# The front of a chunked delta-rule attention reordered ahead of two mixtures of experts

## The chip, the cores and the metric

One core of one Trainium2 chip runs the whole program. The metric is the device time of one execution in microseconds (us); for the kernel before it is 2411.12 us, the median of three runs (2405.57 to 2415.29).

## The reference, cut to what matters

```python
# attention: q, k, v (4, 8, 768, 48), beta (4, 8, 768)
k_n = k / (norm(k, axis=-1) + 1e-6)
for t in range(768):
    y[:, :, t] = einsum('bhd,bhde->bhe', q[:, :, t], state)
    v_old = einsum('bhde,bhd->bhe', state, k_n[:, :, t])
    state = state + beta_t * einsum('bhd,bhe->bhde', k_n[:, :, t], v[:, :, t] - v_old)
x = y.transpose(0, 2, 1, 3).reshape(3072, 384)
# first mixture: 8 experts, all tokens through all of them, weights P
P = exp(x @ w_gate - max); 8 times: rows and columns normalised
out = sum_e P[:, e] * (relu(x @ w1[e]) @ w2[e])     # 384 -> 1024 -> 384
# second mixture: every token goes to one expert, by argmax of normalised scores
```

## The kernel before, in words

The program has three stages on the core: the attention with expert 0 of the first mixture mixed in, experts 1 to 7 of the first mixture over all tokens, and the second mixture over sorted tokens. The change touches only the first stage.

The attention is done in 12 chunks of 64 positions, for 32 heads at once (16 head columns `j` on each half of the partitions, 64 matmuls a product). For each chunk the kernel needs two products that do not depend on the recurrent state: `gram`, keys times keys, and `mix`, keys times queries. ScalarE copies a mix out of PSUM (`copy_m`, L588) and GpSimd masks it (`mask`, L505). VectorE scales a gram by the inverse key norms and beta (`scale`, L858), and SyncE stores it to HBM (`store_a`). The norms come from `kn` loads in six parts of two chunks (`squares_of` L584, `reduce_part` L828, `norms` L835 to L850, done for the first two chunks and then for the other ten).

The triangular inverse of a pair of chunks is solved on VectorE by substitution. `load_blocks(n)` (L339) brings the diagonal 32 by 32 blocks of pair n back from HBM with eight DMAs, `solve` (L876, L879) runs 31 row steps of two instructions, `transpose_blocks` on ScalarE (L595) makes the transpose `sr`, and `store_inverse` (L343, L345) writes `sx` and `sr` to HBM. `load_inverse(c)` (L358, L362, L365) reads them back for chunk c in the layout that TensorE needs, after a wait for those stores.

The recurrence per chunk then runs on TensorE in this order, with ScalarE and VectorE steps between: `cross` (L1224), `corner` (L1232), `write_values` (L1184, psA), `outputs` (L1248, L1184, L1256), `transpose_y` (L1206), `scores` (L1213), and `keys_state` (L1184, psA) for the next chunk. `high_x` (L621, L623) on ScalarE and `low_x` (L513) on GpSimd split the transposed chunk into a high and a low part, `X`. Expert 0 works from these: block k of 96 is `block_hidden(k)` (L1273) and, two steps later, `block_give` (L1290); 8 blocks belong to one chunk.

The order of all this is written out by hand. After a straight prologue every engine runs the same loop over steps s = 0 to 103. Step s holds block s - 8, and lists of step numbers say when each piece of each chunk is issued: `AT_KS`, `AT_X`, `AT_O`, `AT_W`, `AT_Y`, `AT_T`, `AT_SC` for `keys_state`, `cross`, `corner`, `write_values`, `outputs`, `transpose_y` and `scores`; `AT_SOLVED[n]` is the step in which VectorE ends the solve of pair n. From chunk 2 on all lists have a period of 8 steps. In one step TensorE issues its block first, then keys_state, transpose, scores, cross, corner, write_values and outputs, as far as they fall in this step. ScalarE issues the `Relu` of the block (L666), then the copies of the chain, then `high_x`, and only after it `transpose_blocks`. Every engine takes its instructions strictly in this written order. SyncE issues all of the stage's DMAs in one queue, and a wait on it holds everything behind it.

In the kernel before, `cross` of chunk 4 is in step 28, and `AT_SOLVED[2]` is 22:

```python
AT_KS = [None, 4] + [10 + KF * (c - 2) for c in range(2, NC)]
AT_X = [0, 6] + [t + 2 for t in AT_KS[2:]]
AT_T = [t + 1 for t in AT_Y]                      # AT_Y: AT_KS + 7
AT_SOLVED = [None, 7] + [16 * n - 10 for n in range(2, NG)]
```

## Time and profile before

| | before |
|---|---|
| median of 3 runs | 2411.12 us |
| the profiled execution | 2415.61 us |
| its span | 2413.8 us |
| TensorE busy in the span | 93% |
| TensorE busy, us 0 to 203.7 | 104.4 us |
| TensorE busy, us 203.7 to 500 | 295.7 us |
| mean granted clock of TensorE over the span | 0.954 |

The profile page gives for each engine its busy time and share, then the span in 40 slices. In the chain of waits the work that ended last is followed back from the end; the timeline lists instructions with the idle time before them and its releaser. In a windows table a stretch of the span has one row: its length, the busy time of each engine with instruction counts, the granted TensorE clock (1.00 is 2.4 GHz, 0.50 is 1.2 GHz), the busy share of the DMA engines and the rate in GB/s. The stage of the change ends about us 551 of the span; the stages behind it are not edited.

### The profile page before, as it was taken

How to read it: one execution, taken by the hardware profiler on the slowest of the kernel's cores; microseconds unless marked ns; L12 is line 12 of the kernel's file. 1: busy time of each engine (PE TensorE's matmuls, PEld its weight loads, DVE VectorE, ACT ScalarE, POOL GpSimd, SP SyncE). 2: the span in 40 equal slices, each digit the busy share in tenths (PEclk: the TensorE clock that was granted, in tenths of full speed). 3: DMA queues.
4: the chain of work that ended last, by engine and by line, in shares of the span. 5: the costliest groups of instructions: out<-in, count | busy, mean ns of one | idle time of the engine just before them, and what ended most of it. 6: DMA issues, size and time to landing. Idle time of an engine off the chain costs nothing.

```text
span 2413.8 us, 43024 instructions
## 1 busy us (share of the span) xinstructions
PE 2251.8 (93%) x18100; PEld 2089.6 (87%) x18100; DVE 1015.2 (42%) x1787; ACT 611.5 (25%) x1019; POOL 168.4 (7%) x133
## 2 busy tenths in 40 slices
PE   3279999999999999999999999999999996899998
PEld 3279999998999998999899899989999886899998
DVE  4556666335332332323233232333333325666664
ACT  2123333222111111111111111111111122466664
POOL 1231100100000000000000000000000000222221
PEclk7589999999999999999999999999999997899999
DMA  8564443331000000000000000000000012665651
GB/s 233 119 163 104 111 111 90 102 125 46 7 27 1 27 23 5 27 1 27 1 27 27 1 27 1 27 20 8 1 1 1 14 40 63 222 239 201 234 201 61
DMA packets 152487, 166.92 MB, mean 69 GB/s; under 512 B 82956, under 2 KB 113840, under 8 KB 152322
## 3 DMA queue, kind: packets, MB, share of 16 engines
q1 hardware_dynamic: 147458, 152.21, 20.8%
q0 software_dynamic: 4864, 12.20, 1.4%
q8 instruction: 141, 2.31, 0.4%
q14 instruction: 24, 0.20, 0.0%
HBM read 138.42 MB, written 28.71 MB: 69 GB/s over the span
## 4 chain that ended last, share of the span: by engine, by line
PE 91%; DVE 4%; DMA 2%; issue 2%; SPq 1%; ACT 1%; POOL 0%; POOLq 0%; DVEq 0%; ACTq 0%
PE psA L1369 21%; PE psH L1384 15%; PE psB L1369 8%; PE psB L1384 7%; PE psY L1384 7%; PE psY L1478 7%; PE psH L1273 4%; PE psY L1290 4%; PE psA L1465 3%; PE psB L1465 3%; PE psA L1184 3%; PE psB L1256 1%; PE psB L1248 1%; PE psY L1184 1%; DVE products L876 1%
## 5 line engine op out<-in xcount | busy, mean ns | idle before, releaser
L1369 PE MATMUL psA<-X,wh 128*128 128x512 f32 x1440 | 460.5, 401 | 18.1 <-issue 14.0
L1007 DVE SCALAR_TENSOR_TENSOR hl<-psA,hh 128x512 fp32r<-128x512 f32 x240 | 166.0, 692 | 656.6 <-ACT hh L708 656.6
L708 ACT ACTIVATE hh<-psA 128x512 fp32r<-128x512 f32 x240 | 143.8, 599 | 876.9 <-PE psA L1369 876.9
L1369 PEld LDWEIGHTS psA<-X,wh 128*128 128x128 f32 x1440 | 273.8, 193 | 65.9 <-issue 19.7
L1369 PE MATMUL psA<-X,wl 128*128 128x512 f32 x720 | 290.3, 403 | 0.0
L1384 PE MATMUL psH<-wh,hh 128*128 128x384 f32 x672 | 229.0, 341 | 0.0
L1384 PE MATMUL psH<-wh,hl 128*128 128x384 f32 x672 | 227.4, 338 | 0.0
L1384 PE MATMUL psH<-wl,hh 128*128 128x384 f32 x672 | 226.1, 337 | 0.0
L1007 DVE SCALAR_TENSOR_TENSOR hl<-psB,hh 128x512 fp32r<-128x512 f32 x96 | 66.5, 693 | 278.6 <-ACT hh L708 278.6
L1369 PE MATMUL psB<-X,wh 128*128 128x512 f32 x576 | 179.2, 392 | 0.0
L1131 DVE TENSOR_TENSOR vl<-vs,vh 128x768 fp32r<-128x768 f32 x152 | 145.0, 957 | 58.2 <-ACT vh L745 56.6
L1369 PEld LDWEIGHTS psA<-X,wl 128*128 128x128 f32 x720 | 138.5, 192 | 30.3
L708 ACT ACTIVATE hh<-psB 128x512 fp32r<-128x512 f32 x96 | 57.5, 599 | 344.0 <-PE psB L1369 344.0
L745 ACT ACTIVATE vh<-vs 128x768 fp32r<-128x768 f32 x152 | 127.3, 840 | 15.2 <-DMA vs<-v_d 15.2
L1384 PEld LDWEIGHTS psH<-wh,hh 128*128 128x128 f32 x672 | 126.9, 189 | 0.0
L1384 PEld LDWEIGHTS psH<-wl,hh 128*128 128x128 f32 x672 | 126.6, 188 | 0.0
L1384 PEld LDWEIGHTS psH<-wh,hl 128*128 128x128 f32 x672 | 126.2, 188 | 0.0
L1369 PEld LDWEIGHTS psB<-X,wh 128*128 128x128 f32 x576 | 106.7, 188 | 17.7
L1273 PE MATMUL psH<-X,wh 128*128 128x256 f32 x576 | 115.8, 297 | 2.2 <-DVE hlA L886 2.2
L1384 PE MATMUL psB<-wh,hl 128*128 128x384 f32 x336 | 114.4, 341 | 0.0
L1369 PE MATMUL psB<-X,wl 128*128 128x512 f32 x288 | 114.0, 396 | 0.0
L1384 PE MATMUL psB<-wl,hh 128*128 128x384 f32 x336 | 114.0, 339 | 0.0
(236 smaller groups left out, 4290.1 us busy)
## 6 DMA issues: line engine op xcount, KB each, us to landing
vs<-v_d SPq DMA_DIRECT2D x38, 768.0 KB, 6.2
vs<-v_d SPq DMA_DIRECT2D x19, 1536.0 KB, 12.1
ws<-w_d SPq DMA_DIRECT2D x28, 768.0 KB, 6.1
a_scratch<-an SPq DMA_DIRECT2D x12, 512.0 KB, 3.9
kq<-kn_d SPq DMA_DIRECT2D x6, 768.0 KB, 8.6
pk<-kT_d SPq DMA_DIRECT2D x24, 192.0 KB, 4.3
pq<-qT_d SPq DMA_DIRECT2D x24, 192.0 KB, 5.5
vn<-vn_d SPq DMA_DIRECT2D x12, 384.0 KB, 4.5
```

Source lines behind the costliest of these rows:

```text
L708: act.activation(hh[kk % 3][:, :], ps_h[kk % (2 if last else 3)], ACT.Relu).then_inc(hh_ready, 1)
L745: act.activation(piece(to, q), piece(src, q), ACT.Copy).then_inc(vh_ready, 1)
L876: dve.tensor_tensor(pv, sa[n % 2][:, s + 1:BS, s:s + 1].to_broadcast([P, rows, cols]), sx[:, s:s + 1, 0:cols].to_broadcast([P, rows, cols] ...
L1007: dve.scalar_tensor_tensor(hl[b][:, :], ps_h[bank], 0.0, hh[b][:, :].bitcast(F32), ALU.max, ALU.subtract).then_inc(hl_ready, 1)
L1131: dve.tensor_tensor(piece(to, q), piece(src, q), piece(high, q).bitcast(F32), ALU.subtract).then_inc(vl_ready, 1)
L1184: mm = pe.matmul(ps[g * C:g * C + M, j, at:at + W], lhsT[g * C:g * C + K, j, 0:M], rhs[g * C:g * C + K, j, 0:W], start=True, stop=True, sk ...
L1273: mm = pe.matmul(ps_b[k % 2], a[half][:, c, col], X[:, u, b, c, :], start=(n == 0), stop=(n == 3 * KC - 1))
L1290: mm = pe.matmul(ps_u[i], a[k % 4][:, i * P:(i + 1) * P], b[half][:, f % FB, :], start=(f == 0 and n == 0), stop=(f == KF - 1 and n == 2))
L1369: mm = pe.matmul(to, a[half][:, c, col], X[:, 2 * g:2 * g + 2, b, c, :], start=(n == 0), stop=(n == 3 * KC - 1))
L1384: mm = pe.matmul(ps_y[i][:, 0:DM], a[kk % 3][:, q], b[half][:, f, :], start=(f == 0 and n == 0), stop=(f == FB - 1 and n == 2))
L1465: mm = pe.matmul(ps_g[f % 4], a[par][:, c, f * P:(f + 1) * P], b[par][:, c, :], start=(n == 0), stop=(n == 3 * KC - 1))
L1478: mm = pe.matmul(ps_o[s], a[f % 4][:, q], b[par][:, f, :], start=(f == 0 and n == 0), stop=(f == KF - 1 and n == 2))
```

## The change

The edits, all in the first stage:

- Keys and queries for gram and mix are loaded as pairs of chunks (`load_pair`, two DMAs of 48 partitions by two chunks) into three key and three query buffers. All mixes are now done in the prologue; keys of chunks 4 to 11 are loaded a second time for their grams. The keys for chunks 6 and 7 are loaded again after `load_first`, which brings in the first expert's weights.
- The key norms come in three batches: chunks 0 and 1, chunks 2 to 5, chunks 6 to 11.
- The norm of the expert embeddings moves from the start to step 10 (ScalarE) and 11 (VectorE).
- `solve(0)` runs as one uninterrupted stretch on VectorE. On ScalarE all 12 mask copies now stand ahead of `transpose_blocks(0)`.
- Masks, `low_x` and the low half of the first expert's weights move from GpSimd to VectorE; the weights' split moves from the prologue into steps 4 to 9.
- `ts` and `ao` get two buffers; `ao` has its own loader, `load_corner`, and `load_inverse` of both chunks of a pair is issued together.
- The step lists: chunk 1 is done earlier (cross in step 2 and not 6), chunks 2 to 11 are three steps later, `AT_SOLVED` of pairs 2 to 5 is six steps later, pair 1 is solved by step 12 and not 7.

```diff
-AT_KS = [None, 4] + [10 + KF * (c - 2) for c in range(2, NC)]
-AT_X = [0, 6] + [t + 2 for t in AT_KS[2:]]
-AT_W = [2, 8] + [t + 5 for t in AT_KS[2:]]
-AT_Y = [3, 9] + [t + 7 for t in AT_KS[2:]]
+AT_KS = [None, 4] + [13 + KF * (c - 2) for c in range(2, NC)]
+AT_X = [0, 2] + [t + 2 for t in AT_KS[2:]]
+AT_W = [2, 5] + [t + 5 for t in AT_KS[2:]]
+AT_Y = [3, 6] + [t + 7 for t in AT_KS[2:]]
-AT_SOLVED = [None, 7] + [16 * n - 10 for n in range(2, NG)]
+SOLVE_SECOND = [4, 3, 3, 3, 2, 2, 2, 2, 2, 2, 2, 2, 2]
+AT_SOLVED = [None] + [16 * n - 4 for n in range(1, NG)]
+AT_MASK = [None, 2] + [t + 1 for t in AT_KS[2:]]
+AT_SPLIT = {4: (0, 0), 5: (0, 1), 7: (1, 0), 8: (1, 1)}
+AT_EMB = 10
...
# SyncE
+                def load_pair(to, src, m, s):
+                    for g in range(2):
+                        sp.dma_start(to[g * C:g * C + D, :, :, :], src[GR * m:GR * (m + 1), g].rearrange("c d j t -> d c j t")).then_inc(s, 16)
...
-                    for g in range(2):
-                        p0 = g * C + BS
-                        sp.dma_start(aos[p0:p0 + BS, :, :], a_dram[c, p0:p0 + BS, :, 0:BS]).then_inc(s_inv[par], 16)
-                        for k in range(2):
+                    for k in range(2):
+                        for g in range(2):
...
                 load_parts(0)
+                load_pair(kP[0], kT, 0, s_kP[0])
                 sp.dma_start(betas[:, :, :], beta).then_inc(s_beta, 16)
+                load_parts(1)
+                load_pair(qP[0], qT, 0, s_qP[0])
+                load_pair(kP[1], kT, 1, s_kP[1])
+                load_parts(2)
                 sp.dma_start(cst[:, :], consts).then_inc(s_const, 16)
                 sp.dma_start(vns[:, :, :], vn[0]).then_inc(s_vn, 16)
                 for c in range(2):
                     store_a(c)
                 load_blocks(0)
+                sp.wait_ge(s_red, 2)
+                load_pair(qP[1], qT, 1, s_qP[1])
+                load_pair(kP[2], kT, 2, s_kP[2])
+                sp.wait_ge(s_red, 3)
+                load_pair(qP[2], qT, 2, s_qP[2])
+                for m in range(3, PARTS):
                     load_parts(m)
+                for c in range(2):
+                    load_corner(c)
+                store_a(2)
...
+                for m in range(KP, PARTS):
+                    sp.wait_ge(m_done, GR * (m - KP + 1))
+                    if m == KP + 1:
+                        sp.wait_ge(g_done, 4)
+                    load_pair(kP[m % KP], kT, m, s_kP[m % KP])
+                    load_pair(qP[m % KP], qT, m, s_qP[m % KP])
                 sp.dma_start(kns[:, :, :], kn[0]).then_inc(s_kn, 16)
                 halves(kTs, kT, 1, s_kT)
                 halves(qTs, qT, 1, s_qT)
+                sp.wait_ge(m_done, GR * KP + 2)
+                load_pair(kP[0], kT, 2, s_kP[0])
+                store_inverse(0)
+                store_a(3)
+                for c in range(2):
+                    load_inverse(c)
                 load_blocks(1)
+                sp.wait_ge(s_red, PARTS)
+                load_first(0)
+                load_first(1)
+                sp.wait_ge(m_done, NC)
+                load_pair(kP[1], kT, 3, s_kP[1])
+                store_a(4)
+                store_a(5)
                 for s in range(LAST):
+                    if s + 6 < NC:
+                        store_a(s + 6)
+                    if s in (0, 2):
+                        m = 4 + s // 2
+                        sp.wait_ge(g_done, 2 * m - 2)
+                        load_pair(kP[m % 2], kT, m, s_kP[m % 2])
...
-                    if s - 3 in AT_SOLVED:
-                        load_inverse(2 * AT_SOLVED.index(s - 3))
-                    if s - 1 in AT_O[0::2]:
-                        load_inverse(AT_O.index(s - 1) + 1)
+                    if s - 2 in AT_SOLVED:
+                        for par in range(2):
+                            load_inverse(2 * AT_SOLVED.index(s - 2) + par)
+                    if s - 2 in AT_X[0:NC - 2]:
+                        load_corner(AT_X.index(s - 2) + 2)
...
# ScalarE, prologue
                 squares_of(0)
+                root(0)
+                squares_of(1)
+                copy_m(0)
+                squares_of(2)
+                root(1)
+                for c in range(1, 4):
+                    copy_m(c)
+                for c in range(4, NC):
+                    copy_m(c)
+                    if c in (5, 7, 9):
+                        squares_of(3 + (c - 5) // 2)
                 transpose_blocks(0)
+                root(2)
...
# VectorE, prologue
                 reduce_part(0)
+                norms(0)
                 scale(0, psA)
                 scale(1, psB)
+                reduce_part(1)
+                reduce_part(2)
+                norms(1)
+                mask(0)
+                scale(2, psA)
+                solve(0, 0, BS - 1)
+                scale(3, psA)
+                for m in range(3, PARTS):
+                    reduce_part(m)
+                scale(4, psA)
+                scale(5, psH)
+                norms(2)
...
# TensorE, prologue; in step s of the loop then gram(s + 6) after the chain's pieces
                 gram(0, psA)
                 gram(1, psB)
+                mix(0)
                 pe.wait_ge(an_ready, 1)
                 gram(2, psA)
                 pe.wait_ge(an_ready, 2)
+                for c in range(1, 4):
+                    mix(c)
+                pe.wait_ge(an_ready, 3)
+                gram(3, psA)
+                for c in range(4, NC):
+                    mix(c)
+                pe.wait_ge(an_ready, 4)
+                gram(4, psA)
+                pe.wait_ge(mt_copied, NC - 1)
                 gram(5, psH)
```

## Rows read from the trace of the kernel before

**Rows 1.** The page: busy us, share of the span and instructions of each engine.
```profile
PE 2251.8 (93%) x18100; PEld 2089.6 (87%) x18100; DVE 1015.2 (42%) x1787; ACT 611.5 (25%) x1019; POOL 168.4 (7%) x133
```

**Rows 2.** Windows: start:end, length, busy of PE, PEld, DVE, ACT, POOL, clock, DMA.
```profile
0.00:110.90 110.90, 29.39 (x705) 28.80 (x706) 62.41 (x109) 24.61 (x23) 29.05 (x16) 0.64 0.67 178
110.90:176.60 65.70, 51.27 (x1362) 49.64 (x1362) 30.00 (x56) 12.38 (x16) 17.55 (x8) 0.77 0.66 165
176.60:203.70 27.10, 23.70 (x408) 22.59 (x406) 14.30 (x33) 9.16 (x13) 5.61 (x3) 0.87 0.61 155
304.00:500.00 196.00, 195.59 (x3595) 185.31 (x3595) 94.81 (x215) 61.06 (x109) 18.61 (x11) 1.00 0.36 94
```

**Rows 3.** Timeline of the prologue: start, length, engine, line, operation, idle before and releaser.
```profile
22.30 1.47 ACT L584 ACTIVATE kq<-kq 128x1536 f32<-128x1536 f32 x1
90.69 1.94 ACT L595 ACTIVATE sr<-sx 128x1024 f32<-128x1024 f32 x1 [26.04 <-DVE sx L879]
107.74 0.47 SPq L362 DMA_DIRECT2D rs<-r_scratch  x1
110.90 1.92 PE L1224 MATMUL psB<-rs,ao 32*32 32x32 f32 x64 [8.79 <-DMA rs<-r_scratch]
```

**Rows 4.** Windows of short stretches, for the DMA rate and the clock after an idle TensorE.
```profile
3.00:5.00 2.00, 0.00 (x0) 0.00 (x0) 0.00 (x0) 0.00 (x0) 0.00 (x0) 1.00 1.10 402
8.00:12.00 4.00, 4.00 (x94) 4.00 (x92) 0.00 (x0) 0.00 (x0) 0.00 (x0) 1.00 1.04 221
93.00:99.00 6.00, 5.67 (x106) 5.70 (x108) 1.22 (x1) 0.00 (x0) 0.00 (x0) 0.50 1.02 191
555.00:560.00 5.00, 4.79 (x11) 3.80 (x12) 0.06 (x1) 0.58 (x1) 0.00 (x0) 0.50 0.72 212
```

**Rows 5.** Chain of waits in order of time: start, length, piece (step 18 begins at 224.46).
```profile
203.71 1.13 PE psB L1224 x64
224.46 1.27 PE psH L1273 x9
229.09 0.81 PE psB L1206 x6
230.97 1.05 PE psY L1290 x6
235.48 1.13 PE psB L1224 x64
267.25 1.13 PE psB L1224 x64
```

**Rows 6.** Timeline, ScalarE and VectorE, around the inverse of pair 2.
```profile
247.24 2.08 ACT L595 ACTIVATE sr<-sx 128x1024 f32<-128x1024 f32 x1
262.54 0.85 ACT L623 ACTIVATE X<-xf 128x768 fp32r<-128x768 f32 x1
252.64 0.91 DVE L865 MEMSET sx<- 128x1024 f32 x1 [1.89 <-DMA r_scratch<-sr]
```

**Rows 7.** Timeline, SyncE's queue, the same stretch: issue start and length.
```profile
249.34 0.33 SPq L345 DMA_DIRECT2D r_scratch<-sr  x1
249.76 5.71 SPq L339 DMA_DIRECT2D sa<-a_scratch  x8
260.56 0.49 SPq L362 DMA_DIRECT2D rs<-r_scratch  x1
261.09 0.49 SPq L440 DMA_DIRECT2D kn<-kn_d  x1
261.62 0.90 SPq L318 DMA_DIRECT2D qT<-qT_d  x2
262.56 0.88 SPq L318 DMA_DIRECT2D kT<-kT_d  x2
```

**Rows 8.** The solve's tile: count, ns min/median/max of one, start of the first and last.
```profile
L876 DVE TENSOR_TENSOR products<-sa,sx x186: 190/361/2439, 39.6 to 433.2; 128x31 f32<-128x31 f32 x12, 128x60 f32<-128x60 f32 x12, 128x87 f32<-128x87 f32 x12, 128x112 f32<-128x112 f32 x12
L879 DVE TENSOR_TENSOR sx<-sx,products x186: 191/374/1773, 39.8 to 433.4; 128x31 f32<-128x31 f32 x12, 128x60 f32<-128x60 f32 x12, 128x87 f32<-128x87 f32 x12, 128x112 f32<-128x112 f32 x12
```

More of the change, by code:

```diff
@@ L27 @@
 PARTS = 6
-KQ = 4
+BATCH_ENDS = [1, 3, PARTS]
+KP = 3
+NA = 3
 E, F = 8, 1024
@@ L71, in solve_plan @@
     plan, done = {}, 0
-    for s in range(8):
-        n = min(4, BS - 1 - done)
-        plan[s] = (1, done, done + n)
-        done += n
+    for s, k in enumerate(SOLVE_SECOND):
+        plan[s] = (1, done, done + k)
+        done += k
     for n in range(2, NG):
@@ L136, in build @@
         end_dense = top[0]
-        kq = [keep(f"kq{i}", [P, 2 * NJ, D], at=w_at + 4 * 2 * NJ * D * i) for i in range(KQ)]
+        part, pair = 4 * 2 * NJ * D, 4 * GR * NJ * C
+        kq = [keep(f"kq{i}", [P, 2 * NJ, D], at=w_at + i * part) for i in range(PARTS)]
+        qP = [keep(f"qP{i}", [P, GR, NJ, C], at=at) for i, at in enumerate((wl_at + 2 * part, w_at, w_at + pair))]
         fh1 = [keep(f"fh1_{i}", [P, KC, FH], at=wl_at + 4 * KC * FH * i) for i in range(2)]
@@ L153, in build @@
         rs = [keep(f"rs{i}", [P, NJ, C]) for i in range(2)]
-        ts, aos, xx = keep("ts", [P, NJ, BS]), keep("ao", [P, NJ, BS]), keep("xx", [P, NJ, BS])
+        ts, aos = [keep(f"ts{i}", [P, NJ, BS]) for i in range(2)], [keep(f"ao{i}", [P, NJ, BS]) for i in range(2)]
+        xx = keep("xx", [P, NJ, BS])
         zz, ww, st = keep("zz", [P, NJ, D]), keep("ww", [P, NJ, D]), keep("st", [P, NJ, D])
@@ L243, in build @@
         sx_init, sol, sr_ready, inv_out = sem("sx_init"), sem("sol"), sem("sr_ready"), sem("inv_out")
+        s_ao = [sem(f"s_ao{i}") for i in range(2)]
         x_done, x_ready, o_done, r_ready = sem("x_done"), sem("x_ready"), sem("o_done"), sem("r_ready")
@@ L961, in _ @@
                         state(AT_Y.index(s - 1))
+                    if s - 1 in AT_T:
+                        low_x(AT_T.index(s - 1))
                     u = unit_after(s)
@@ L1253, in outputs @@
                     pe.wait_ge(mt_ready, c + 1)
+                    if c == 0:
+                        pe.wait_ge(r_ready, 4)
                     for g, j in heads():
```

297 lines of the change are left out of this document (130 added, 167 removed).

## The prediction

> **What bounds the kernel now.** I read the page first: TensorE is busy for 93% of the span, and no other engine for half of it [rows 1]. The windows say where the other 7% lies that this change can reach. From us 304 to 500, inside the loop, TensorE is busy 195.6 of 196.0 us at full clock; up to us 203.7 it is busy only 104.4 us in three windows, much of it at the low clock (means 0.64, 0.77, 0.87) [rows 2]. So there are two regimes. In the front TensorE waits, and what counts is the chain through DMAs, VectorE and ScalarE. From the second chunk on TensorE sets the end alone: whatever it idles there is added to the time in full, and nothing taken from another engine there is worth anything. I therefore compare one landmark, `cross(2)`, which starts at 203.71 [rows 5], and then ask whether the loop behind it stays free of waits.
>
> The timeline of the prologue shows the old chain: the first squares start at 22.3, because ScalarE stood at the expert embeddings, which are queued behind all the first loads; the solve of pair 0 ends when `sr` starts at 90.7; the last inverse load is issued at 107.7 and `cross(0)` starts at 110.9 [rows 3].
>
> **The front, part by part.** All times are my placement of the new order, with durations of the rows.
>
> *DMA.* A load to all 128 partitions ran at 402 GB/s, one to 48 partitions (keys and queries) at 221, both at a full busy share [rows 4]. The prologue now brings twelve pair loads (0.79 MB each, 3.6 us at 221: 43 us), six norm parts (12 us at 402), three gram stores, eight small block loads, constants and values (some 10 us together) before the last mix can run. With a start of 2.3 us and some 4 us of waits for buffers that is us 71.5 for the last queries. From them: two mixes at the low clock, since TensorE idles before each pair (106 matmuls took 5.67 us there [rows 4], so 64 take 3.4 to 3.7): 79; the copy out of PSUM about 1: 80. The transpose stands behind copy 11 on ScalarE, though the solve ended long before: the blocks are back at 29.5, and 31 steps of 0.36 + 0.37 us [rows 8] make 23 us: 52.6. The clean solve thus gives nothing here; it is the mixes and their loads that are late next. `sr` 1.9 us: 82; its store lands 3.3 us after issue [rows 6, 7]: 85; six loads issued in 3.2 us, the last lands some 3 us after its issue (cross(0) began 3.2 us after it before [rows 3]): `cross(0)` at 91, 20 us earlier than now.
>
> *Behind it* SyncE issues six more inverse loads and eight block loads (8 us), the expert weights (2 us of issue, 3.15 MB, 8.3 us of transfer) and only then the keys of chunks 6 and 7, which move behind the weights in the same queue: they land at 110.5. `gram(6)` stands directly behind `cross(0)` on TensorE, so TensorE idles 17 us there. Half of the gain is gone by this one place.
>
> *Steps 0 to 7* hold six grams, the rest of chunk 0 and all of chunk 1. Before, us 110.9 to 176.6 held the same but seven mixes more and without the last three pieces of chunk 1: 51.3 us busy at a mean clock of 0.77 [rows 2], 39.5 at full clock, less seven mixes of 1.9, plus 8 us for those pieces (a period of 31.8 us less eight blocks leaves 13.2 for a chunk's chain [rows 5]): 34 us of TensorE, 6 us more for two stretches at the low clock, and 9 us of waits (chunk 8's keys behind the store of gram 6: 1; `keys_state(1)` behind `scale(9)` and solve steps on VectorE: 5; write values and scores of chunk 0: 3). The first block starts at 110.5 + 49 = 159.5.
>
> *Steps 8 to 12.* VectorE has ten solve steps, five `low`, half the weight split, `low_x` and the embedding norm: some 15 us against 11 on TensorE. The solve of pair 1 ends at 177.4; `sr` 2.1, store 3.3 (182.7), three issues more and six inverse loads: `cross(2)` at 191.7, after 9 us of idle TensorE. Masks, `low_x` and split on VectorE cost 0 beyond this: GpSimd did them off the path, and in the loop VectorE is busy 95 of 196 us [rows 2]; if that cover were gone, a mask (1.2 us) would be late by its own length.
>
> So cross(2) moves from 203.7 to 191.7: 12.0 us. It also has three more blocks behind it, step 15 and not 12, each 1.27 + 1.05 us [rows 5]: 7.0. **The front gains 19 us.**
>
> **The loop, and what falls due in it.** `AT_SOLVED` moves six steps, the crosses three. Before, pair 2 was solved in step 22 and crossed in 28; now it is 28 and 31. I lay the chain on the clock of step 29, t = 0 at its start. Step 29 is also `AT_T[3]`. In the old order the same three steps are 18 to 20: they start at 224.46, the transpose ends at 229.90, so t = 5.4, and `cross` starts at 235.48, t = 11.0 [rows 5]. ScalarE issues `high_x(3)` before `transpose_blocks(2)`: `xf` and `X` after the transpose end 7.2 us after the step's start (262.54 + 0.85 [rows 6] against 224.46 and a period of 31.77, 256.2). Then:
>
> - `sr`, 2.08 us: 9.3. Its store is issued and lands 3.3 us later (249.34 to 252.64): 12.6 [rows 6, 7].
> - SyncE issues the eight block loads of pair 4 (5.71), then `kn`, `qT`, `kT` (0.49, 0.90, 0.88), all ahead of the inverse loads [rows 7]: 17.9.
> - Six inverse loads, 2.8 to 3.5 us to the issue of the last, 2.5 to land: 23.2 to 23.9.
>
> TensorE stands at `cross(4)` from 11.0: **12.5 us idle**. The same for pair 3. Pairs 4 and 5 have no block loads ahead, and wait for the store to land (12.6) instead: 12.6 + 2.9 + 2.5 = 18.0, **7 us idle** each. Nothing covers this: cross is ahead of the next block in TensorE's order, and the next blocks are ready. Before, the same chain ended with the last load landing at 260.56 + 2.5 = 263.1 against the cross at 267.25 [rows 5, 7]: 4.2 us of slack with six steps' distance, so three steps' distance cannot do. Sum: 2 x 12.5 + 2 x 7 = 39 us.
>
> After an idle stretch the granted clock is 0.50, that is 1.2 GHz, and work goes at half pace: fully so from 93 to 99 after a long wait, and from 555 to 560 after 4 us [rows 4]. Some 6 us at half pace are 3 us lost, five times (pairs 1 to 5): 15 us.
>
> **Sum.** -19 + 39 + 15 = +35 us. The profiled execution took 2415.6 us with a span of 2413.8; with the change 2450.6. It lies 4.5 us above the median of the runs, so the prediction is 2411.1 + 35 = 2446 us. Unknown sizes: the front's 19 may be 5 (each of steps 0 to 7 at the low clock, late weights) to 30; the loop's 39 may be 32 to 46; the clock's 15, 8 to 18 (the row after 4 us of idle shows only 5 us). That is +15 to +55: 2426 to 2466.
>
> **Rivals.**
>
> *The inverse arrives in time* (faster). If ScalarE or SyncE run the pair's chain ahead of TensorE, for instance because the transposes or the loads pass where I see them held, only the front's 19 us are left and perhaps 3 at pair 1: 2411 - 19 = 2392. For it: VectorE has the solve ready before step 29 starts. Against: `high_x(3)` waits for a transpose of the same step, and the slack now is only 4.2 us at twice the distance. It decides from a landing at t = 11 or less, and I find 18 at best. 0.17.
>
> *Pair loads run at the full rate.* The 48-partition rate is the rate of two chunks' pieces of 192 KB; one larger DMA might go at 402. Then each pair takes 2.0 and not 3.6 us, 12 pairs and the late keys 21 us less, of which buffers and half clocks keep 3: +35 - 18 = +17, 2428. Against: these small loads already fill the DMA engines' time, with a busy share of 1.04 [rows 4]. 0.12. The Trainium skill (DMA: Bandwidth & Descriptors, Anatomy of one DMA) gives a DMA a fixed 2.0 us and then bytes by 436 GB/s, which is this rival; the same skill (SBUF — State Buffer, Door 1: The DMA port swizzle) lets 64 partitions in a row reach only half the ports. This trace's 221 against 402 GB/s agrees with the second and not with the first.
>
> *The front gives nothing* (slower still). If the wait at `gram(6)` and the extra VectorE work make cross(2) no earlier than 203.7 less the 7 us of blocks, the gain is 7 or less and the loop's loss stays: +47 to +55, about 2463. For it: 3.15 MB are moved in front of a load on the path. Against: cross(0) at 91 leaves 20 us to spend. 0.13.
>
> **How the numbers follow.** Forecast 0.58 (2426 to 2466), in time 0.17, full rate 0.12, no front 0.13. What can be told from no change is 0.5%, 12 us. Faster by more than that: the first rival, with part of the forecast's low end, 0.18. Within: 0.10. Slower: 0.72. The range runs from 2402 to 2474: it leaves out most of the first rival and the far end of the last, under 0.2 together.
>
> **What would show it.** cross(0) near 91 and cross(2) near 192; gram(6) released by a DMA of keys near 110; in the waits table TensorE L1224 waiting for a DMA of `rs` from `r_scratch` five times, 7 to 13 us each, the two longest for pairs 2 and 3; ScalarE's `sr` directly behind an `X` there; windows of clock 0.50 behind each. If those waits are absent, the prediction is wrong at its root; if cross(2) is after 203, its front is.

## The result and the profile after

The changed kernel takes 2467.94 us (median of four runs, 2462.66 to 2474.41); the kernel before, run beside it, 2412.23 (four runs, 2405.57 to 2415.29). The ratio is 1.0236, 95% interval 1.0203 to 1.0269: slower by 56 us, where 35 were forecast. The profiled span is 2472.5 us against 2413.8, that is +58.7, and the mean granted clock 0.941 against 0.954.

The page after, in its first line (busy us, share, instructions), answers to [rows 1]:

```profile
PE 2280.5 (92%) x18100; PEld 2117.9 (86%) x18100; DVE 1016.1 (41%) x1823; ACT 613.8 (25%) x1020; POOL 106.4 (4%) x106
```

TensorE runs as many instructions in 29 us more of busy time: part of the loss is work at the lower clock. VectorE took over GpSimd's work and is no busier than it was. The windows of the kernel after (columns as in [rows 2]) are cut at its own landmarks: `cross(0)`, the first block, `cross(2)`, and the same inner stretch as before.

```profile
0.00:107.30 107.30, 56.79 (x1153) 55.45 (x1154) 46.53 (x97) 24.84 (x24) 3.55 (x8) 0.70 0.93 201
107.30:191.60 84.30, 56.20 (x1177) 54.56 (x1177) 33.52 (x64) 12.35 (x16) 1.47 (x1) 0.55 0.60 150
191.60:222.50 30.90, 19.47 (x189) 18.05 (x188) 19.09 (x48) 10.01 (x16) 2.16 (x1) 0.90 0.48 117
304.00:500.00 196.00, 165.89 (x2915) 157.35 (x2915) 95.81 (x225) 48.99 (x86) 8.13 (x5) 0.89 0.34 81
```

`cross(0)` comes 3.6 us earlier than before, the first block 15.0 us later, `cross(2)` 18.7 us later. Each of these starts is read from one execution. e8 below has the first stage of the kernel before, unchanged, and there the three start at 108.0, 174.5 and 200.1 and not at 110.9, 176.6 and 203.7, so a difference of some 3 us in them says nothing: the gain at `cross(0)` is not clear of this, the two losses are. The stretch from 304 to 500, full before [rows 2], now has 30 us of idle TensorE and a clock of 0.89. The timeline of the front (start, length, engine, line, operation, idle before and its releaser) answers to [rows 3]:

```profile
36.66 16.54 SPq L366 DMA_DIRECT2D ao<-a_scratch  x4
57.47 0.93 SPq L329 DMA_DIRECT2D kP<-kT_d  x2
70.06 3.68 PE L1235 MATMUL psH<-qP,kP 48*64 48x64 f32 x64 [12.05 <-issue]
107.30 1.92 PE L1284 MATMUL psB<-rs,ao 32*32 32x32 f32 x64 [2.60 <-issue]
129.50 3.68 PE L1235 MATMUL psA<-kP 48*64 48x64 f32 x64 [20.28 <-DMA kP<-kT_d]
222.46 1.92 PE L1284 MATMUL psB<-rs,ao 32*32 32x32 f32 x64 [8.62 <-DMA rs<-r_scratch]
```

The row at 70.06 is mix 6, the one at 129.50 `gram(6)`. How full the DMA engines were ahead of it, in windows of the kernel after (columns as in [rows 2]; the last two figures are their busy share and the rate in GB/s), with one window behind it, for the clock:

```profile
0.00:89.00 89.00, 44.21 (x896) 43.11 (x896) 41.09 (x90) 20.71 (x20) 3.55 (x8) 0.70 0.95 203
60.00:70.00 10.00, 0.00 (x0) 0.00 (x0) 1.75 (x1) 0.46 (x1) 0.00 (x0) 0.50 1.02 181
70.00:80.00 10.00, 7.75 (x157) 7.68 (x159) 0.61 (x1) 3.42 (x3) 0.00 (x0) 0.67 1.03 171
130.00:140.00 10.00, 10.00 (x242) 9.70 (x240) 5.46 (x13) 1.18 (x2) 0.00 (x0) 0.50 0.53 136
```

The loop's waits, from the table of waits (engine, line, awaited thing; us in all, times, longest):

```profile
PE psB L1284 <- DMA rs<-r_scratch: 51.9, 5, 13.4
PE psY L1353 <- DVE y0s L928: 10.4, 8, 2.0
```

and the same table of the kernel before:

```profile
PE psA L1369 <- issue: 14.0, 4, 3.8
PE psB L1224 <- DMA rs<-r_scratch: 8.8, 1, 8.8
```

Before, TensorE waited once for an inverse, at `cross(0)` [rows 3], and at no later cross; now it waits at `cross(2)`, (4), (6), (8) and (10), as forecast: 8.6, 13.4, 13.1, 8.4 and 8.3 us. The stall at `cross(4)`, in the timeline of SyncE, ScalarE and TensorE (columns as above), answers to [rows 6, 7]:

```profile
287.72 0.81 ACT L641 ACTIVATE xf<-psB 128x768 f32<-128x768 f32 x1 [3.47 <-PE psB L1263]
288.56 0.85 ACT L643 ACTIVATE X<-xf 128x768 fp32r<-128x768 f32 x1
289.31 2.00 ACT L611 ACTIVATE sr<-sx 128x1024 f32<-128x1024 f32 x1
291.34 0.32 SPq L357 DMA_DIRECT2D r_scratch<-sr  x1
291.76 4.59 SPq L351 DMA_DIRECT2D sa<-a_scratch  x8
297.86 0.89 SPq L321 DMA_DIRECT2D kT<-kT_d  x2
298.86 0.36 SPq L380 DMA_DIRECT2D rs<-r_scratch  x1
300.85 3.31 SPq L380 DMA_DIRECT2D rs<-r_scratch  x1
306.66 1.92 PE L1284 MATMUL psB<-rs,ao 32*32 32x32 f32 x64 [13.39 <-DMA rs<-r_scratch]
```

Read it as a queue: `sr` stands behind `xf` and `X`, the store behind `sr`, eight block loads and three more transfers behind the store, and only then the inverse. The windows behind it show the price of the clock: 12 us at 0.50 (1.2 GHz) around the stall, then 0.99 (2.4 GHz).

```profile
300.00:312.00 12.00, 5.34 (x78) 5.28 (x79) 0.72 (x3) 1.56 (x3) 0.32 (x1) 0.50 0.91 161
312.00:314.00 2.00, 2.00 (x71) 1.71 (x70) 1.82 (x3) 0.35 (x1) 1.16 (x1) 0.99 0.10 14
```

**The account of the span.** +18.7 us at `cross(2)`. From there to the first product of expert 1 (555.2 before, 636.2 after) +62.3: the four stalls 43.2, the `y0s` waits 10.4, and a rest of 8.7, which is what remains of the half-clock work when the seven us of blocks that already lie ahead of `cross(2)` are taken off. From there to the end -22.3. That last term has nothing to do with attention: no instruction of it was edited.

### The profile page after: what moved, and what is told of

Read it like the earlier page. It is cut to its first block, busy times and chain, and to the rows that moved or that the text cites. A ratio compares the mean times of both kernels' runs of the same rounds, so it can differ in the third digit from the quotient of the medians.

```text
span 2472.5 us, 43060 instructions
## 1 busy us (share of the span) xinstructions
PE 2280.5 (92%) x18100; PEld 2117.9 (86%) x18100; DVE 1016.1 (41%) x1823; ACT 613.8 (25%) x1020; POOL 106.4 (4%) x106
## 4 chain that ended last, share of the span: by engine, by line
PE 85%; DVE 6%; SPq 4%; DMA 2%; issue 2%; ACT 1%; POOL 0%; POOLq 0%; DVEq 0%; ACTq 0%
PE psA L1427 20%; PE psH L1442 14%; PE psB L1427 8%; PE psB L1442 7%; PE psY L1442 7%; PE psY L1536 6%; PE psA L1523 3%; PE psB L1523 3%; PE psA L1235 3%; PE psH L1338 3%; PE psY L1353 3%; PE psH L1235 1%; DVE products L906 1%; PE psB L1311 1%; DVE sx L909 1%
```

## The experiments

Each batch had its own runs of the kernel before; ratios are against those. The medians before differ by up to 2 us between batches, so a difference of two medians of different batches can be off by as much. "Block" and "expert" are the starts, in the profile, of the first block product and of the first product of expert 1.

| Kernel | Median us | Ratio, 95% interval | Block | Expert |
|---|---|---|---|---|
| before | 2412.2 to 2414.2 | 1 | 176.6 | 555.2 |
| after | 2467.94 | 1.0236 [1.0203, 1.0269] | 191.6 | 636.2 |
| e1 before, inverse late | 2464.95 | 1.0218 [1.0199, 1.0238] | 175.9 | 607.9 |
| e2 after, inverse early | 2427.41 | 1.0068 [1.0044, 1.0091] | 190.2 | 589.0 |
| e3 after, keys first | 2463.18 | 1.0198 [1.0177, 1.0219] | 187.0 | 627.2 |
| e5 after, single loads | 2466.09 | 1.0220 [1.0203, 1.0237] | 189.2 | 626.6 |
| e4 after, queues cleared | 2421.30 | 1.0037 [1.0020, 1.0054] | 190.9 | 583.9 |
| e6 after, corner later | 2476.61 | 1.0272 [1.0250, 1.0294] | 192.1 | 635.5 |
| e7 after, four repairs | 2413.06 | 1.0009 [0.9992, 1.0027] | 186.4 | 573.2 |
| e8 before, code shifted | 2391.24 | 0.9917 [0.9895, 0.9938] | 174.5 | 553.2 |
| e9 after, masks on GpSimd | 2481.84 | 1.0285 [1.0263, 1.0307] | 191.2 | 643.0 |
| e10 after, corners late | 2465.22 | 1.0212 [1.0191, 1.0234] | 186.9 | 628.1 |
| e11 e8, inverse first | 2392.55 | 0.9918 [0.9898, 0.9938] | 172.9 | 552.3 |
| e12 e7 varied | 2420.29 | 1.0031 [1.0016, 1.0047] | 182.1 | 576.4 |

**e1: the stalls alone, put into the kernel before.**

```diff
-AT_SOLVED = [None, 7] + [16 * n - 10 for n in range(2, NG)]
+AT_SOLVED = [None, 7] + [16 * n - 7 for n in range(2, NG)]
-                    if s - 3 in AT_SOLVED:
+                    if s - (3 if s < 12 else 2) in AT_SOLVED:
...
```

> The kernel before with one part of the change alone: pairs 2 to 5 are solved three steps before their cross (AT_SOLVED 16n - 7) and their inverse is read one step before it; front, engines of the masks and all else stay as before. Theory (the distance in steps is what costs): TensorE L1224 waits for rs from r_scratch four times, about 13, 13, 8 and 8 us, with 3 us of half-speed work behind each, so the kernel is 48 to 56 us slower than the kernel before: about 2463. Rival (the loop's loss after the change comes from VectorE's added masks and low_x, or from the pair-wise inverse loads): the kernel stays within 5 us of 2412.

Measured 2464.95, 50.8 us above the kernel before of its batch. The table of waits:

```profile
PE psB L1224 <- DMA rs<-r_scratch: 56.9, 5, 14.9
PE psA L1369 <- issue: 14.5, 4, 3.9
```

One of the five waits, 8.0 us, is the old one at `cross(0)`; the late hand-over makes the other four, 14.9, 14.2, 9.9 and 9.9 us, 48.9 in all, and with them nearly as much loss as the whole change brings, without anything of the new front. It keeps the 14.5 us of "issue" gaps, which become e8's question.

**e2: the stalls taken out of the changed kernel.**

```diff
-AT_SOLVED = [None] + [16 * n - 4 for n in range(1, NG)]
+AT_SOLVED = [None, 12] + [16 * n - 6 for n in range(2, NG)]
```

> The changed kernel with AT_SOLVED of pairs 2 to 5 two steps earlier (16n - 6 in place of 16n - 4), nothing else. Theory: the four waits of 7 to 13 us at cross (43.2 us in the trace) go but for a few us, and with them four stretches of half-speed work (3 us each): 2468 - 52 = about 2416, with the wait of 8.6 us at cross(2) left, and the eight waits of 1.3 us for y0s left. Rival (VectorE is too busy in the loop with masks, low_x and solve): solving earlier only moves the wait to hlA, and the time falls by less than 20 us.

Measured 2427.41, 40.5 us less than the changed kernel:

```profile
PE psY L1353 <- DVE y0s L928: 12.3, 8, 2.4
PE psB L1284 <- DMA rs<-r_scratch: 8.3, 1, 8.3
PE psB L1284 <- DVE pm L1023: 6.2, 7, 1.7
```

All four stalls are gone and `cross(2)` keeps its own. Eleven us of the forecast didn't come: half of that is a small new wait at `cross`, for VectorE's copy of the scores. In VectorE's order that copy stands behind solve steps and the mask. At chunk 3 the mask took 2.17 us, against 1.22 in the changed kernel; how much of the wait is due to the mask and how much to the solve steps was not separated.

**e3: the keys of chunk 6 ahead of the blocks and the expert's weights.**

```diff
+                sp.wait_ge(m_done, NC)
+                load_pair(kP[1], kT, 3, s_kP[1])
                 load_blocks(1)
                 sp.wait_ge(s_red, PARTS)
                 load_first(0)
                 load_first(1)
-                sp.wait_ge(m_done, NC)
-                load_pair(kP[1], kT, 3, s_kP[1])
```

> The changed kernel with the keys of chunks 6 and 7 loaded before the blocks of pair 1 and the first expert's weights, nothing else. Theory (gram(6) waits for keys queued behind 3.15 MB of weights): gram(6) starts near 116 and not at 129.5, and since TensorE waits in that stretch, 8 to 13 us come off: about 2457. Rival (the weights or the blocks of pair 1, now later, are the next to be late, at solve(1) or at the first block): under 4 us.

Measured 2463.18, 5 us less than the changed kernel (9 by the ratios), below the forecast, and within the width of the two intervals. TensorE's timeline says why:

```profile
116.70 3.68 PE L1235 MATMUL psA<-kP 48*64 48x64 f32 x64 [7.10 <-DMA kP<-kT_d]
138.70 3.57 PE L1235 MATMUL psH<-kP 48*64 48x64 f32 x62 [7.35 <-DMA kP<-kT_d]
```

`gram(6)` comes at 116.7 and not at 129.5, as forecast; but the weights now stand ahead of chunk 8's keys, and a wait of 7.35 us appears there that the changed kernel did not have.

**e5: each pair load split into single-chunk loads.**

```diff
-                        sp.dma_start(to[g * C:g * C + D, :, :, :], src[GR * m:GR * (m + 1), g].rearrange("c d j t -> d c j t")).then_inc(s, 16)
+                        for i in range(GR):
+                            sp.dma_start(to[g * C:g * C + D, i, :, :], src[GR * m + i, g]).then_inc(s, 16)
...
```

> The changed kernel with each pair load issued as four DMAs of one chunk's 48 partitions (192 KB) as in the kernel before, in place of two of 384 KB; same bytes, order and waits. Theory (the rate is set by 48 partitions, not by the size of the DMA): the last mix ends within 3 us of 95.3 and the time stays within 4 us of the changed kernel's 2468. Rival (the pair form itself is slow, since 60 to 90 us moved only 171 to 194 GB/s against 221 before): the mixes end 10 us or more earlier and so does the kernel.

Measured 2466.09: no difference from the changed kernel that these runs can tell. Loading in pairs neither speeds nor slows the front.

**e4: the order of the inverse's chain in the two queues.** SyncE issues both chunks' inverse loads directly behind the store, ScalarE transposes the solved blocks before it splits X.

```diff
                         store_inverse(n)
+                        for par in range(2):
+                            load_inverse(2 * n + par)
                         if n + 2 < NG:
                             load_blocks(n + 2)
...
-                    if s - 2 in AT_SOLVED:
-                        for par in range(2):
-                            load_inverse(2 * AT_SOLVED.index(s - 2) + par)
...
-                    if s in AT_T:
-                        high_x(AT_T.index(s))
                     if s - 1 in AT_SOLVED:
                         transpose_blocks(AT_SOLVED.index(s - 1))
+                    if s in AT_T:
+                        high_x(AT_T.index(s))
```

> The changed kernel with the pair chain's queueing taken out: SyncE issues both chunks' loads of the inverse directly behind the r store, ahead of that step's weight blocks, and ScalarE copies the step's transposed block before it splits the chunk's X. If the four waits of cross(4), (6), (8), (10) (43.2 us in the changed kernel) come from work queued ahead on SyncE and ScalarE, they shrink to 1 to 3 us each and the time falls 30 to 45 us to about 2430. If they come from the chain itself, solved 3 steps too late for its DMA round trip, the inverse loads alone save only 2 to 4 us a pair, and the time falls 8 to 15 us.

Measured 2421.30, 46.6 us less, a little beyond the good end of the forecast. This edit also acts on pair 1, whose wait falls from 8.6 to 4.0 us. Timeline of pair 2 in this kernel, to be laid beside the fence of the kernel after:

```profile
278.77 2.02 ACT L610 ACTIVATE sr<-sx 128x1024 f32<-128x1024 f32 x1
280.81 0.32 SPq L357 DMA_DIRECT2D r_scratch<-sr  x1
282.34 0.81 ACT L640 ACTIVATE xf<-psB 128x768 f32<-128x768 f32 x1 [1.55 <-PE psB L1262]
285.06 0.33 SPq L380 DMA_DIRECT2D rs<-r_scratch  x1
290.01 1.92 PE L1283 MATMUL psB<-rs,ao 32*32 32x32 f32 x64 [2.12 <-DMA rs<-r_scratch]
```

The stall falls from 13.39 to 2.12 us, and the three parts of the 11.3 can be read off. Against `xf`, `sr` starts 3.6 us earlier and not 1.6 later: 5.2 from ScalarE's order. From the store to the first inverse load 4.25 us and not 7.5: 3.3 from SyncE's, and what is left is the store's own landing. From that issue to `cross(4)` 4.95 and not 7.8: 2.85 from loads that no longer stand at their issue (the 3.31 us above). So three steps' distance is almost enough where nothing stands ahead of the chain.

**e6: the corner one step later.**

```diff
-AT_O = [1, 3] + [t + 3 for t in AT_KS[2:]]
+AT_O = [1, 3] + [t + 4 for t in AT_KS[2:]]
```

> The changed kernel with the corner block of each pair one step later, so that step 17 (and every eighth after it) has chain work again between a unit's hidden products and the next unit's first output product. If the 10.4 us of TensorE's waits for y0s (8 waits of 1.3 us, none before the change) come from that empty step, they go, and the time falls 8 to 10 us to about 2458. If they come from VectorE's larger load (masks and low parts), they stay, and the time stays within 3 us.

Measured 2476.61, a miss: not faster, and if anything slower. The `y0s` waits fall only to 7.9 us in four, and 3.0 us of waits of no named releaser stand in their place. e7 and e12 come back to them.

**e7: four repairs together.** e2 (two steps earlier, not three as the expectation has it), e3, e6, and for pair 1 the inverse loads ahead of the block loads:

```diff
                         store_inverse(n)
                         if n + 2 < NG:
+                            if n == 1:
+                                for par in range(2):
+                                    load_inverse(2 * n + par)
                             load_blocks(n + 2)
...
```

> The changed kernel with four repairs together: the solve handed over three steps earlier (16n-6, pair 1 at step 12), the corner one step later, the keys of chunk 6 ahead of the first step's blocks, pair 1's inverse loads ahead of that step's blocks. By the single results (41, 8 to 10, 5, and up to 8 of the 8.3 us that cross(2) still waits) the time is 2400 to 2412, which would bring it level with the kernel before; if the repairs overlap (cross(2) is then bound by its chain of products and the clock), 2415 to 2425.

Measured 2413.06 (1.0009 [0.9992, 1.0027]): level with the kernel before, no better, and between the two forecasts. `cross(2)` starts at 212.69 with a wait of 4.18 us; the first block is still 10 us later than before, and expert 1 starts 18 us later. The total is level only because this kernel has the shorter experts' loop that e8 is about; against e8, the kernel before with that loop, it is 22 us slower.

**e8: TensorE's code moved by sixteen instructions.** In the kernel before:

```diff
+                for _ in range(16):
+                    pe.wait_ge(s_const, 16)
                 with pe.Fori(2, E - 1) as e:
```

> The kernel before with 16 further TensorE waits, all long satisfied, between the blocks and the experts' loop: nothing but the place of the loop's instructions in TensorE's code moves. In the kernel before TensorE stands 3.2 to 3.8 us in every turn of that loop, waiting for nothing that the profile shows (14.0 us in four turns), each time with half-clock work behind it; in the changed kernel these gaps are 1.6 us in all. If the place of the code sets them, they change in size or go, and the time falls up to 22 us to about 2392. If something in the data or in the DMA traffic at that time sets them, they stay at 3 to 4 us each, and the time stays within 3 us of the kernel before.

Measured 2391.24, ratio 0.9917 [0.9895, 0.9938]: 21 us faster than the kernel before, as forecast, and 77 us faster than the changed one. One of the gaps in question, in the timeline of the kernel before:

```profile
961.52 1.22 PE L1369 MATMUL psA<-X,wh 128*128 128x512 f32 x2 [3.77 <-issue]
```

and its group after the shift:

```profile
L1369 PE MATMUL psA<-X,wh 128*128 128x512 f32 x1440 | 455.1, 397 | 6.6 <-DVE wl L1000 4.1 <-issue 2.4
```

The idle time of no named releaser in this group falls from 14.0 to 2.4 us. The windows over the experts' loop give its full price, gaps and the half-clock work behind them. Kernel before:

```profile
555.20:2021.30 1466.10, 1446.63 (x7211) 1307.68 (x7212) 473.55 (x759) 248.19 (x401) 0.80 (x2) 0.98 0.05 16
```

With the shift:

```profile
553.20:1996.10 1442.90, 1434.65 (x7210) 1297.96 (x7211) 473.21 (x759) 247.68 (x401) 0.80 (x2) 0.99 0.05 17
```

23.2 us less for the same products. In the changed kernel the loop takes 1443.8 (636.2 to 2080.0), with 1.6 us of such gaps: it got this gain by the way, since its edits also moved TensorE's code. e8 shows that the place of the code alone can bring such a gain; that the -22.3 of the account has the same cause is a conclusion from the same gaps missing and the same length of loop. All fourteen kernels agree with it: the gaps sum to 14.0 us before and 14.5 in e1, whose code of TensorE is that of the kernel before, and to 0.9 to 2.4 in the other twelve; from the first product of expert 1 to the end of the span it is 1858.6 and 1856.1 us in those two and 1835.7 to 1840.7 in the rest. That it is the fetching of instructions at the loop's turn fits (the page's row of the instruction queue has 141 packets in those two and 137 in all others), but was not shown.

**e9: masks and low parts back on GpSimd**, at the same steps.

```diff
-                def mask(c):
-                    dve.wait_ge(mt_copied, c + 1)
-                    dve.tensor_tensor(mt[c][:, :, :], mt[c][:, :, :], later.unsqueeze(1).to_broadcast([P, NJ, C]), ALU.mult).then_inc(mt_ready, 1)
...
+                def mask(c):
+                    pool.wait_ge(mt_copied, c + 1)
+                    pool.tensor_tensor(mt[c][:, :, :], mt[c][:, :, :], later.unsqueeze(1).to_broadcast([P, NJ, C]), ALU.mult).then_inc(mt_ready, 1)
```

> The changed kernel with the masks and the low parts of X back on GpSimd, at the same steps; the split of the first expert's weights and the embedding norm stay on VectorE. If those twelve masks and twelve low parts lie beside TensorE's work (the prediction's value, 0), the time stays within 3 us of the changed kernel. If they make VectorE late for the copy-outs y0s, the 10 us of TensorE's waits for y0s go and the time falls 8 to 12 us; the corner one step later did not remove them, so one of these two must be so.

Measured 2481.84, 14 us more than the changed kernel (12 by the ratios, 8.5 in the profiled spans): both expectations miss. GpSimd's timeline in the loop:

```profile
338.67 1.85 POOL L538 TENSOR_TENSOR X<-xf,X 128x768 fp32r<-128x768 f32 x1 [24.78 <-ACT X L657]
340.47 2.56 POOL L534 TENSOR_TENSOR mt<-mt,cst 128x1024 f32<-128x1024 f32 x1
```

and VectorE's at the same time:

```profile
338.42 0.42 DVE L923 TENSOR_TENSOR sx<-sx,products 128x252 f32<-128x252 f32 x1
338.88 1.92 DVE L920 TENSOR_TENSOR products<-sa,sx 128x255 f32<-128x255 f32 x1
340.83 2.49 DVE L923 TENSOR_TENSOR sx<-sx,products 128x255 f32<-128x255 f32 x1
```

Two solve instructions of about 0.42 us take 1.92 and 2.49: each ends 0.3 us after the GpSimd instruction that runs beside it. They are lengthened by 1.50 and 2.07 us, where doing GpSimd's work itself costs VectorE 0.96 and 1.22. The Trainium skill (SBUF — State Buffer, SBUF: two separate sides) has the two engines lock a shared pair of ports against each other, when the VectorE instruction has two SBUF inputs and the GpSimd instruction reads SBUF, and whichever starts first holds it to its end; this trace agrees with it.

But this is not where the 8.5 us lie. The crosses of the loop start as in the changed kernel, the last of them, `cross(11)`, at 580.8 against 581.8. From there to expert 1 it takes 62.3 us and not 54.5, and these 7.8 us fall together with the reduction over partitions that begins the gating, GpSimd's first after its masks and low parts. In e9:

```profile
604.92 1.81 POOL L538 TENSOR_TENSOR X<-xf,X 128x768 fp32r<-128x768 f32 x1 [23.70 <-ACT X L657]
616.26 0.38 POOL L563 PARTITION_ALL_REDUCE gmax<-gmax  x1 [9.54 <-issue]
```

In the changed kernel it starts at 608.20, released by VectorE's input. GpSimd stands 9.54 us between its last low part and this reduction, for nothing that the profile names; the kernel before has the same gap, 8.8 us. VectorE waits 6.8 us for it, then ScalarE, and TensorE for both (2.9 and 1.7 us, with work at 1.2 GHz behind); that this is the whole of the 7.8 is read from these waits and was not tested. So what the move to VectorE gained in this execution is at the end of the stage, and in the loop it cost nothing and gained nothing that shows. What the gap consists of was not tested. The `y0s` waits stay, 8.4 us in eight: these masks and low parts on VectorE are not their cause.

**e10: the corner loads behind the pair loads.**

```diff
                 for m in range(3, PARTS):
                     load_parts(m)
-                for c in range(2):
-                    load_corner(c)
-                store_a(2)
...
                 for m in range(KP, PARTS):
...
+                for c in range(2):
+                    load_corner(c)
+                store_a(2)
```

> The changed kernel with the four corner loads, the store of gram 2 and three small loads issued behind the key and query loads of pairs 3, 4 and 5, not ahead of them. In the changed kernel SyncE stands 16.5 us at the corner loads, while mixes 0 and 1, which free the buffer of pair 3, are done at 46.2; the loads of pair 3 are issued at 57.5. If the order of issue made the last mixes late, mix 6 starts up to 11 us before 70.1, cross(0) comes 6 to 11 us before 107.3, and the time falls 5 to 10 us. If the DMA queue was full at that time, so that any load stands there as long, mix 6 comes at most 4 us earlier and the time falls 0 to 3 us.

Measured 2465.22, 2.7 us less (6 by the ratios), inside the intervals. The timeline of SyncE and TensorE:

```profile
59.59 15.03 SPq L366 DMA_DIRECT2D ao<-a_scratch  x4
64.74 3.68 PE L1235 MATMUL psH<-qP,kP 48*64 48x64 f32 x64 [6.97 <-issue]
```

Mix 6 comes 5.3 us earlier and `cross(0)`, at 102.06, 5.2: between the two theories. The expectation has one premise wrong: pair 3's buffer is free when mix 1 ends, at 29.2 in the changed kernel, and not at 46.2, which is the end of mix 3. So the new order issued the loads of pair 3 at 34.4 and not at 57.5, 23 us earlier, and only 5 of these reached mix 6. The corner loads stand nearly as long in their new place. Both say that the DMA engines were full and that the order of issue was the smaller part. At `gram(6)` the wait stays 21 us, and the 5 us reach the first block (186.9).

**e11: e8, with chunk 2's inverse loads ahead of the block loads.**

```diff
                         store_inverse(n)
+                        if n == 1:
+                            load_inverse(2)
                         if n + 2 < NG:
                             load_blocks(n + 2)
...
```

> The kernel before with the 16 satisfied TensorE waits ahead of the experts' loop (2391 by the last runs) and, for pair 1, chunk 2's inverse loads directly behind the r store, ahead of the block loads of pair 3. If the 8.8 us that TensorE waits for rs at cross(2) come from the eight block loads ahead of them on SyncE, 5 to 8 us of the wait go and the time is 2384 to 2387. If cross(2) is held by the solve itself, the wait and the time stay as they are, 2391.

Measured 2392.55 against 2391.24: nothing. The question was put at the wrong place. The 8.8 us are the wait at `cross(0)` [rows 3]; it is 9.1 in e8 and 6.8 here, in code that the edit does not touch. `cross(2)` had no wait to lose. In e8 and here:

```profile
200.10 1.20 PE L1224 MATMUL psB<-rs,ao 32*32 32x32 f32 x64
199.76 1.20 PE L1226 MATMUL psB<-rs,ao 32*32 32x32 f32 x64
```

Neither row has idle time before it. The loads of the inverse are issued by 193.6 in e8 and by 189.0 here, and neither kernel needed them sooner. So e11 says nothing of what holds `cross(2)`, neither for the block loads nor for the solve.

**e12: the repairs once more**, with e10's order of the loads and without e6's corner step; the diff is the second difference from e7.

```diff
-AT_O = [1, 3] + [t + 4 for t in AT_KS[2:]]
+AT_O = [1, 3] + [t + 3 for t in AT_KS[2:]]
```

> The changed kernel with all repairs that helped: the solve handed over three steps earlier, pair 1's inverse loads ahead of the block loads, the keys of chunk 6 ahead of the first step's blocks, the corner loads behind the pair loads; the corner stays at its own step. From the version with the corner one step later (2413): 0 to 8 us for the corner, and 3 us for the order of the loads alone, more if the keys' place now lets cross(0)'s 5 us pass on: 2402 to 2410, 0.1 to 0.5% below the kernel before. If the front is bound by the transfers as a whole, the two changes of order cancel, and it stays at 2410 to 2415.

Measured 2420.29 (1.0031 [1.0016, 1.0047]), a miss, and above e7. The waits for `y0s` in e7:

```profile
PE psY L1356 <- DVE y0s L931: 4.8, 4, 1.7
```

and in e12:

```profile
PE psY L1356 <- DVE y0s L931: 11.9, 8, 2.1
```

From the first block to the first product of expert 1 it is 386.8 us in e7 and 394.3 in e12. e12 reaches the first block 4.3 us earlier by its order of loads and loses 7.5 us behind it. The two kernels differ in the order of the front's loads and in the corner's step, and the loss is nearly the 7.1 us of `y0s` waits; so with the stalls gone, the corner's step is taken to be worth that much. In e6, with the stalls there, it bought nothing (`cross(2)` to expert 1 takes 412.6 us, 413.8 in the changed kernel). Why it fails beside the stalls stays open. e12 beats neither kernel; e8 beats both.

## Why the prediction was right in kind and 21 us short

By its own steps, against the profiled span (+58.7; +35 forecast). Every measured figure is of one execution:

| Step | Forecast | Measured | Off |
|---|---|---|---|
| `cross(0)` | 91 | 107.3 | +16.3 |
| wait at `gram(6)` and its start | 17; 110.5 | 20.3; 129.5 | +2.7 |
| steps 0 to 7, to the first block | 49 | 62.1 | +13.1 |
| first block to `cross(2)` | 32.2 | 30.9 | -1.3 |
| four stalls, pairs 2 to 5 | 39 | 43.2 | +4.2 |
| half clock behind the stalls, less 7.0 of blocks (measured: what remains) | 8 | 8.7 | +0.7 |
| waits for `y0s` | none | 10.4 | +10.4 |
| experts' loop | none | -22.3 | -22.3 |

The sum of the last column is 23.8, and 35 + 23.8 is the measured 58.7 but for rounding.

*The stalls: right, and shown three ways.* Four of them put into the kernel before cost 51 us with their clock (e1), the four taken out of the changed one give 41 (e2), and the order of the two queues, which acts on pair 1 too, gives 47 (e4). The prediction's chain also had the right members: `sr` behind `xf` and `X`, the loads behind the blocks and `kn`, `qT`, `kT`. What was too small: the third inverse load stood 3.3 us in SyncE's queue, and pairs 4 and 5 waited some 8 us each and not 7.

*The front: the step that failed.* It is the sum that ends in "us 71.5 for the last queries". The last mix ended at 95.3 where 79 was forecast, and from there to `cross(0)` it took 12.0 us, just as forecast: all of the 16.3 lies ahead of the last mix. The sum had 65 us of transfers and 6 us in which the DMA engines stood. Up to us 89 they were busy 95% of the time, so the 6 us were about right, and the transfers themselves took some 20 us more. The price of the pair loads is the term that can be named: 221 GB/s came from one window of 4 us [rows 4], and where almost nothing but such loads ran, from 60 to 80, the rate was 181 and then 171 at a full busy share. By these rates the twelve pairs (9.4 MB) take an estimated 54 us and not 43, about half of the 20; the rest was not separated. Why the same kind of load ran slower there is open; e5 shows only that it is not the form of the pair loads. The written order played a smaller part. SyncE stood 16.5 us at the corner loads, so that pair 3 was issued at 57.5 though its buffer was free at 29.2; e10 takes this away and gains 5 us. The solve of pair 0 was late as well, since the gram stores issued at 16.0 landed at 28.0 and only then the eight block loads could go, but it ended at 58.4, long before the mixes.

*Steps 0 to 7: mis-sized by the clock.* They were forecast with 40 us of TensorE, two short stretches of it at the low clock, and 9 us of waits. From `gram(6)` to the first block TensorE was busy 54.3 us and idle 7.8, at a mean clock of 0.57. From 130 to 140 it was busy 10.0 of 10.0 us and had a granted clock of 0.50 all the while, and the same from 140 to 150: the forecast's "Some 6 us at half pace" behind an idle stretch did not hold here. The wait at `gram(6)` was right in place and size; e3 shows why it can't simply be moved.

*Masks, `low_x`, split: "cost 0".* For masks and `low_x` in the loop the 0 was right in size, though "GpSimd did them off the path" was not the whole of it: with them on GpSimd, solve instructions of VectorE are stretched from 0.42 to 1.92 and 2.49 us, yet the last cross starts within 1 us of the same place (e9). At the end of the stage it was wrong in sign: there the move spares the gap of 9.5 us ahead of GpSimd's first reduction, and the execution with the gap came 7.8 us later to expert 1. The rows of the solve carried a hint of the stretching: maxima of 2439 and 1773 ns beside medians of 361 and 374 [rows 8]. A row whose maximum is five times its median asks what ran beside it. The split of the weights was not tested by itself.

*The waits for `y0s`: not seen.* Moving the chain by three steps left steps 17, 25, ... without a chain piece between a block's hidden products and a unit's first output product, which waits for the previous unit's copy out of PSUM. With the stalls away, filling the step took the waits from 11.9 to 4.8 us (e12 to e7); beside the stalls it did not (e6), so this cause is shown only in part. The prediction counted what was late in the chain and not what the chain had covered.

*The experts' loop: not seen, and of the opposite sign.* The rows of 555 to 560 at clock 0.50 were read as a price of idling; the four "issue" gaps in the table of waits of the kernel before were not asked about, although 14 us with no named releaser was its third-largest wait. Without this gift the changed kernel would have stood some 78 us above and outside the range given. That the total came so near was luck, for misses of opposite sign offset each other: +30.8 us up to `cross(2)` and +10.4 for `y0s` against -22.3.

*The rivals.* The inverse did not arrive in time (five waits). The pair loads did not run at the full rate but below the lower one (171 to 181 GB/s). The third rival, a front that gives nothing, is what happened, and more so: `cross(2)` 18.7 us later than before. The formula with 436 GB/s that the prediction takes from the Trainium skill (DMA: Bandwidth & Descriptors, Anatomy of one DMA) is given there for DMAs that GpSimd issues; these are issued by SyncE.

## What to carry to other kernels

When a producer is moved nearer to its consumer, write out every queue on its way, in order, with the work that stands ahead in that very step: here the order in two queues was worth 47 us, and with them clear the three steps' distance left waits of only 4.7 us in pairs 2 to 5. Before a sum of transfers is built on a rate, read that rate in more than one window of the same kind of load: 221 GB/s in one, 171 in another, cost this forecast more than the order of issue. And before an experiment on a wait, find the instruction that waits: the table gives a line, and one line is twelve crosses (e11). When a chain piece is moved away from a step, ask what it covered there. Before any work inside a loop, look for idle time whose releaser is "issue" at the loop's turn: here moving the code by sixteen instructions was worth 21 us.

## What the runs showed of the hardware

- TensorE stood 3.2 to 3.9 us at each of four turns of its loop over experts, for no wait that the profile names, in the kernel before and e1 (14.0 and 14.5 us in all), and 0.9 to 2.4 us in all in the twelve kernels whose code lies elsewhere. Sixteen instructions ahead of the loop (e8) took it from 1466.1 to 1442.9 us.
- SyncE stood 16.54 us at the issue of four small loads behind some MB of others, and 15.03 us when they were issued later (e10); one small load in the loop stood 3.31 us and another 0.36.
- Loads to 48 partitions ran at 221 GB/s in one window and at 181 and 171 in others, each time with the DMA engines' busy share above 1.
- Two VectorE instructions of 0.42 us took 1.92 and 2.49 us beside GpSimd's of 1.85 and 2.56 (e9).
- GpSimd stood 8.8 us (before) and 9.54 us (e9) between its last ordinary instruction and its first reduction over partitions, for nothing that the profile names. Where it had been idle for 50 us ahead of the reduction, as in the changed kernel, no such gap shows.
- TensorE was busy 10.0 of 10.0 us from 130 to 140 at a granted clock of 0.50.
